# Attention and squared-ReLU MLP in one kernel: the softmax sums of three batches taken by block transposes and additions on VectorE, the last keys' product with v as two column tiles, and the second group of scores beside it

## The chip, the cores and the metric

The kernel runs on one core of one Trainium2 chip. The metric is the device time of one execution in microseconds (us), the median of several runs.

## The reference

Attention over q, k, v of shape (4 batches, 12 heads, 448 positions, 64), all float32, with capped scores, and then an MLP over the 4 x 448 tokens of width 768.

```python
scores = cap * np.tanh(scale * (q @ k.T) / cap)
attn = np.exp(scores - max);  attn = attn / (np.sum(attn, axis=-1, keepdims=True) + 1e-09)
x = (attn @ v).transpose(0, 2, 1, 3).reshape(4 * 448, 768)
h = x @ w_in                      # w_in (768, 2048)
r = np.maximum(h, 0.0)
g = s * (r * r) + b
y = g @ w_out                     # w_out (2048, 768)
```

## The kernel before

Work goes by pairs of heads: 24 pairs, six to a batch (PAIRS = 6, ALL = 24). For a pair everything is kept transposed, keys on the 128 partitions and the 448 queries along the free dimension. 448 keys are three full tiles of 128 (FULL = 3) and 64 left over. The left-over keys of both heads share one tile (AB): head 0 in its lower 64 partitions, head 1 in its upper ones. So e, the exponentials of a pair, is 7 tiles of 128x448.

TensorE, for a pair p: `first_scores(p)` makes four score tiles by four matmuls with 64 rows each (L249, two heads side by side as row tiles); `last_scores(p)` makes the AB tile by one whole-array matmul with a block-diagonal k (L258) and two row tiles (L261). `values(p)` multiplies e with v: first the AB tile with a block-diagonal v as one whole-array matmul that starts the accumulation (L272), then six matmuls of 64 output columns each (L277, column tiles, head 0 into PSUM partitions 0 to 63 and head 1 into 64 to 127). `sums(p)` multiplies the sum of the e tiles with a tile of ones, one column tile a head (L287): every partition of a head's half then holds that head's sum over keys. All these products are plain float32; the profile counts two records a matmul.

ScalarE makes e with `first_tanh`, `exponential`, `last_tanh`, `exponential` (L374 to L385). VectorE's `add_e(p)` adds the 7 tiles into e_sum (L465 to L472; two operations of 128x896 and two of 64x448). Its `scale_pair(p)` then waits for `sums(p)`, transposes the sums from PSUM in blocks of 32x32 (L479), adds the guard to one column a block (L481), inverts 14 numbers a partition (L484), spreads them back by a second block transpose (L486), multiplies with the product of `values(p)` (L490), and splits the result into a high and a low part (L495, L497), since the MLP's products run as three fp32r matmuls each (hi x hi, lo x hi, hi x lo).

There are three stages. First stage, pairs 0 to 5 (batch 0): attention only; TensorE runs `first_scores(p+1)`, `values(p)`, `last_scores(p+1)`, `sums(p)`. Two PSUM tensors, pv and hid, take turns (`pv_bank`). Second stage, periods 6 to 23: in period p TensorE does the scores of pair p+1, the values and sums of pair p, and between them 16 chunks (SHARE = 16) of the first MLP product of the batch before. A chunk (`hidden_chunk`, L306 to L308) is three matmuls; six chunks make one of 16 tiles of 128x448 in one of the two banks of hid. The order in a period is: first scores, 6 chunks, last scores, 2 chunks, values, sums, 8 chunks. Both values and sums of every pair use pv (bank 0 and bank 1). A tile is rectified by ScalarE (`rectify`, L395) into one of three slots of hidden_sb, squared by VectorE (`square`, L503), and stored by a DMA of queue SP (L182); rectify waits for the store three tiles before. Third stage: the last batch's first product and then all of the second product, `out_products`, L320 to L322; hidden tiles come back by DMA.

The weights w_in arrive in 24 pieces of 256 KB into a ring of four slots (`work`), each cast to fp32r by VectorE (`w_in_high`, L457) and its rest subtracted by GpSimd (L580). Twelve pieces are cast in the first stage, and three in each of periods 6 to 9. SP issues the loads of a period in program order with the stores and the loads of v and of q and k, and waits in that order too.

Of the kernel before, what the change touches and what calls it, by code (L numbers as in the profile page):

```python
# [7 lines left out]
ACT = mybir.ActivationFunctionType  # L8

# [26 lines left out]
BLOCK = 32  # L36
QK_SLOTS = 3
# [5 lines left out]
def attention_ffn(nc, q_k, v, cap, w_in, w_out, s, b, y_t):  # L43
    hidden = nc.dram_tensor("hidden_scratch", (B - 1, JT, P, S), F32).ap()
    ctx = ExitStack()
    with ctx:
# [20 lines left out]
        turned = sb("turned", [P, S], F32)  # L67
        r_sum = sb("r_sum", [P, S], F32)
        xt = sb("xt", [P, S], F32)
        recips = sb("recips", [P, 2, S // BLOCK], F32)  # L70
# [41 lines left out]
        sums_read = sem("sums_read")  # L112
        recip_done = sem("recip_done")
# [17 lines left out]
        def pv_bank(p):  # L131

            return hid if p < PAIRS and p % 2 else pv
# [22 lines left out]
        def _(sp):  # L156
# [46 lines left out]
            for p in range(PAIRS, ALL):  # L203
# [36 lines left out]
        def _(pe):  # L240
# [24 lines left out]
            def values(p):  # L265
                i, of = p % QK_SLOTS, p % 2
                out = pv_bank(p)
# [3 lines left out]
                reach(pe, x_done, p - 1 if p < PAIRS else p)  # L271
                nc.tensor.matmul(out[:, 0, 0:S], v_sb[:, i, 2 * FULL * D:], e[:, of, AB, :], start=True, stop=False)  # L272
                for t in range(FULL):
                    for head in range(2):
                        rows = slice(head * D, (head + 1) * D)
                        tile = (head * FULL + t) * D
                        last = nc.tensor.matmul(out[rows, 0, 0:S], v_sb[:, i, tile:tile + D], e[:, of, 2 * t + head, :],  # L277
                                                start=False, stop=t == FULL - 1)
                last.then_inc(pv_done, 1)

            def sums(p):
                out = pv_bank(p)
                pe.wait_ge(e_sum_done, 4 * (p + 1))
                reach(pe, sums_read, p - 1 if p < PAIRS else p)
# [54 lines left out]
            for p in range(PAIRS, ALL):  # L339
# [27 lines left out]
        def _(act):  # L367
# [51 lines left out]
            for p in range(PAIRS, ALL):  # L419
# [4 lines left out]
                for j in tiles_in(SHARE * c, SHARE * c + 6):  # L424
                    rectify((batch - 1) * JT + j)
# [3 lines left out]
                for j in tiles_in(SHARE * c + 6, SHARE * (c + 1)):  # L429
                    rectify((batch - 1) * JT + j)  # L430
# [22 lines left out]
        def _(dve):  # L453
# [7 lines left out]
            def add_e(p):  # L461
                of = p % 2
                dve.wait_ge(exp_done, 2 * p + 1)
                reach(dve, sums_done, p)
                nc.vector.tensor_tensor(e_sum[:], e[:, of, 0:2, :], e[:, of, 2:4, :], ALU.add).then_inc(e_sum_done, 1)  # L465
# [8 lines left out]

            def scale_pair(p):
                batch, c = divmod(p, PAIRS)
                out = pv_bank(p)
                dve.wait_ge(sums_done, p + 1)
                nc.vector.transpose(turned[:], out[:, 1, 0:S]).then_inc(sums_read, 1)  # L479
                dve.wait_ge(sums_read, p + 1)  # L480
                nc.vector.tensor_scalar(recips[:, 0, :], turned[:].rearrange("p (n i) -> p n i", i=BLOCK)[:, :, 0],  # L481
                                        guard_c, None, ALU.add).then_inc(recip_done, 1)
                dve.wait_ge(recip_done, 3 * p + 1)
                nc.vector.reciprocal(recips[:, 1, :], recips[:, 0, :]).then_inc(recip_done, 1)  # L484
                dve.wait_ge(recip_done, 3 * p + 2)
                nc.vector.transpose(r_sum[:], recips[:, 1, :].unsqueeze(2).broadcast_to([P, S // BLOCK, BLOCK])  # L486
# [123 lines left out]
```

## Time and profile before

| | |
|---|---|
| median of 3 runs | 677.98 us (677.97 to 678.04) |
| profiled execution | 678.0 us, span 676.2 us |
| TensorE busy | 663.9 us, 98% |
| VectorE busy | 282.3 us, 42% |
| ScalarE busy | 246.5 us, 36% |
| GpSimd busy | 33.4 us, 5% |
| granted TensorE clock | 1.00 (full, 2.4 GHz) |

The span runs from the first to the last instruction; the rest of the time lies around it. Busy time of TensorE counts a matmul until its modelled end, so a busy engine can still pass from one shape to another with small gaps: starts are the better measure. Idle time of an engine other than the one that sets the end costs nothing by itself.

### The profile page before, as it was taken

The page shows a single profiled execution, that of the slowest core. Times are in us where ns is not written, and L with a number is a line of the kernel's source. Part 1 is how long each engine was busy: PE and PEld are TensorE (multiplying, and loading weights), DVE is VectorE, ACT ScalarE, POOL GpSimd, SP SyncE. Part 2 cuts the span into 40 slices and gives each one's busy share as a digit, 9 for nine tenths or more (in the row PEclk, how much of TensorE's full clock was granted, in tenths as well). Part 3 has the DMA queues.
Part 4 walks back from the last instruction along what each step waited for, and adds up shares of the span by engine and source line. Part 5 has one row for each costly group of instructions (what it writes and reads, how often), then busy time and mean ns, then how long its engine had stood idle before and what let it go on. Part 6 is the DMA issues. An engine that isn't in the chain of part 4 may idle for free.

```text
span 676.2 us, 7857 instructions
## 1 busy us (share of the span) xinstructions
PE 663.9 (98%) x3122; PEld 500.0 (74%) x3122; DVE 282.3 (42%) x449; ACT 246.5 (36%) x255; POOL 33.4 (5%) x32
## 2 busy tenths in 40 slices
PE   7998999999999999999999999999999999999998
PEld 4332666666666666666667799999999999999997
DVE  3798744644445545545445343322431222212211
ACT  5777444444444444434442133222331121112110
POOL 2331222200000000000000000000000000000000
PEclk9999999999999999999999999999999999999999
DMA  7542134313213212221310331123152224215002
GB/s 221 167 142 91 44 103 145 100 57 98 83 57 98 83 57 85 86 67 47 100 51 36 118 94 47 50 68 113 31 190 69 59 77 138 56 41 178 1 0 82
DMA packets 38100, 57.93 MB, mean 86 GB/s; under 512 B 11440, under 2 KB 29872, under 8 KB 38064
## 3 DMA queue, kind: packets, MB, share of 16 engines
q1 hardware_dynamic: 37632, 57.43, 27.3%
q8 instruction: 25, 0.41, 0.3%
q14 instruction: 11, 0.09, 0.0%
q10 hardware_dynamic: 432, 0.00, 0.0%
HBM read 40.90 MB, written 16.52 MB: 85 GB/s over the span
## 4 chain that ended last, share of the span: by engine, by line
PE 96%; DVE 2%; ACT 1%; DMA 1%; issue 0%; SPq 0%; DVEq 0%
PE hid L306 13%; PE hid L307 12%; PE hid L308 12%; PE scores L321 8%; PE scores L320 8%; PE scores L322 8%; PE pv L277 7%; PE scores L249 6%; PE pv L321 4%; PE pv L322 4%; PE pv L320 4%; PE scores L261 3%; PE scores L258 3%; PE pv L272 2%; PE pv L287 2%; ACT e L379 1%
## 5 line engine op out<-in xcount | busy, mean ns | idle before, releaser
L306 PE MATMUL hid<-x_hi,w_hi 128*128 128x448 f32 x384 | 146.2, 381 | 0.6 <-DVE xt L490 0.6
L307 PE MATMUL hid<-x_lo,w_hi 128*128 128x448 f32 x384 | 140.5, 366 | 0.0
L308 PE MATMUL hid<-x_hi,w_lo 128*128 128x448 f32 x384 | 140.5, 366 | 0.0
L306 PEld LDWEIGHTS hid<-x_hi,w_hi 128*128 128x128 f32 x384 | 72.0, 188 | 40.8 <-issue 34.2
L320 PE MATMUL scores<-x_hi,w_hi 128*128 128x448 f32 x256 | 93.5, 365 | 0.0
L321 PE MATMUL scores<-x_lo,w_hi 128*128 128x448 f32 x256 | 93.5, 365 | 0.0
L322 PE MATMUL scores<-x_hi,w_lo 128*128 128x448 f32 x256 | 93.5, 365 | 0.0
L385 ACT ACTIVATE e<-e,const 128x1792 f32<-128x1792 f32 (+1 forms) x48 | 77.0, 1604 | 1.6
L308 PEld LDWEIGHTS hid<-x_hi,w_lo 128*128 128x128 f32 x384 | 72.1, 188 | 6.4
L307 PEld LDWEIGHTS hid<-x_lo,w_hi 128*128 128x128 f32 x384 | 72.2, 188 | 5.4
L508 DVE SCALAR_TENSOR_TENSOR x_lo<-e,const,x_hi 128x448 fp32r<-128x448 f32 x48 | 32.1, 683 | 103.8 <-ACT x_hi L399 103.8
L399 ACT ACTIVATE x_hi<-e,const 128x448 fp32r<-128x448 f32 x48 | 31.3, 669 | 104.5 <-PE pv L322 104.5
L395 ACT ACTIVATE hidden_sb<-hid 128x448 f32<-128x448 f32 x48 | 25.8, 537 | 117.8 <-PE hid L308 117.8
L374 ACT ACTIVATE e<-scores,const 128x1792 f32<-128x1792 f32 x24 | 42.2, 1758 | 44.4 <-PE scores L249 44.4
L479 DVE STREAM_TRANSPOSE turned<-pv 128x448 f32<-128x448 f32 x21 | 13.7, 651 | 95.2 <-PE pv L287 95.2
L277 PE MATMUL pv<-e,v_sb 128*64 128x448 f32 x252 | 52.0, 548 | 0.0
L320 PEld LDWEIGHTS scores<-x_hi,w_hi 128*128 128x128 f32 x256 | 48.1, 188 | 3.8
L321 PEld LDWEIGHTS scores<-x_lo,w_hi 128*128 128x128 f32 x256 | 48.1, 188 | 3.8
L322 PEld LDWEIGHTS scores<-x_hi,w_lo 128*128 128x128 f32 x256 | 48.1, 188 | 3.8
L503 DVE SCALAR_TENSOR_TENSOR hidden_sb<-hidden_sb,const 128x448 f32<-128x448 f32 x48 | 31.8, 683 | 44.8 <-ACT hidden_sb L395 44.3
L249 PE MATMUL scores<-qk 64*128 64x448 f32 x192 | 42.6, 561 | 5.1 <-ACT e L379 4.8
L320 PE MATMUL pv<-x_hi,w_hi 128*128 128x448 f32 x128 | 46.7, 365 | 0.0
(63 smaller groups left out, 658.4 us busy)
## 6 DMA issues: line engine op xcount, KB each, us to landing
qk<-q_k SPq DMA_DIRECT2D x24, 448.0 KB, 3.3
hidden_scratch<-hidden_sb SPq DMA_DIRECT2D x48, 224.0 KB, 1.9
e<-hidden_scratch SPq DMA_DIRECT2D x48, 224.0 KB, 2.6
work<-w_in SPq DMA_DIRECT2D x24, 256.0 KB, 4.1
e<-w_out SPq DMA_DIRECT2D x16, 384.0 KB, 3.1
y_t<-qk SPq DMA_DIRECT2D x24, 224.0 KB, 2.0
v_sb<-v SPq DMA_DIRECT2D x24, 192.0 KB, 2.5
k_ab<-q_k SPq DMA_DIRECT2D x48, 16.0 KB, 3.1
```

Source lines behind the costliest of these rows:

```text
L249: last = nc.tensor.matmul(scores[:, 2 * t + head, 0:S], qk[rows, i, 1, t * P:(t + 1) * P], qk[rows, i, 0, :], start=True, stop=True)
L277: last = nc.tensor.matmul(out[rows, 0, 0:S], v_sb[:, i, tile:tile + D], e[:, of, 2 * t + head, :], start=False, stop=t == FULL - 1)
L306: nc.tensor.matmul(out, w_hi[:, j, w], x_hi[:, batch % 2, c, :], start=c == 0, stop=False)
L307: nc.tensor.matmul(out, w_hi[:, j, w], x_lo[:, batch % 2, c, :], start=False, stop=False)
L308: last = nc.tensor.matmul(out, w_lo[:, j, w], x_hi[:, batch % 2, c, :], start=False, stop=c == CT - 1)
L320: nc.tensor.matmul(y_acc(c), w_hi[:, j, w], ring(x_hi, n), start=j == 0, stop=False)
L321: nc.tensor.matmul(y_acc(c), w_hi[:, j, w], ring(x_lo, n), start=False, stop=False)
L322: last = nc.tensor.matmul(y_acc(c), w_lo[:, j, w], ring(x_hi, n), start=False, stop=j == JT - 1)
L374: nc.scalar.activation(e[:, of, 0:G1, :], scores[:, 0:G1, 0:S], ACT.Tanh, scale=tanh_scale).then_inc(tanh_done, 1)
L385: nc.scalar.activation(e[:, p % 2, tiles, :], e[:, p % 2, tiles, :], ACT.Exp, scale=cap_c).then_inc(exp_done, 1)
L503: nc.vector.scalar_tensor_tensor(r, r, s_c, r, ALU.mult, ALU.mult).then_inc(sq_done, 1)
L508: nc.vector.scalar_tensor_tensor(ring(x_lo, n), source, b_c, ring(x_hi, n).bitcast(F32), ALU.add, ALU.subtract).then_inc(g_lo_done, 1)
```

## The change

In the second stage the sums are no longer a matmul. VectorE transposes e_sum in blocks of 32x32 (128x896), sums each block's 32 elements (a reduction to 28 numbers a partition), brings the four groups of 32 partitions beside each other by one guarded addition and three copies, sums those, inverts, copies the results back to four groups of partitions, and spreads them by a last block transpose as before. `invert(p)` for pair p stands a period earlier than the multiplication, behind `scale_pair(p-1)`. The first stage keeps the matmuls with ones (`invert_first`). In all pairs the AB tile's product with v becomes two column tiles (64 columns of the block-diagonal v each, all 128 rows), last in `values`, so that the whole-array matmul is gone. In the second stage the products of successive pairs take turns on the two banks of pv, and `values(p)` waits for x of pair p-1. The order in a period becomes: first scores, 8 chunks, last scores, values, 8 chunks. `add_e` is cut in two, the first addition standing before the squares. SP issues the loads of v and of q and k ahead of the period's stores.

```diff
         def pv_out(p):
+            return first_banks(p)[:, 0, 0:S] if p < PAIRS else pv[:, p % 2, 0:S]
...
@@ sync, period p
-                for j in tiles_in(SHARE * c, SHARE * c + 8):
-                    store_hidden((batch - 1) * JT + j)
                 if p + 2 < ALL:
                     load_v(p + 2)
-                for j in tiles_in(SHARE * c + 8, SHARE * (c + 1)):
-                    store_hidden((batch - 1) * JT + j)
                 if p + 3 < ALL:
                     load_qk(p + 3)
+                for j in tiles_in(SHARE * c, SHARE * (c + 1)):
+                    store_hidden((batch - 1) * JT + j)
...
@@ tensor, values(p)
-                reach(pe, x_done, p - 1 if p < PAIRS else p)
-                nc.tensor.matmul(out[:, 0, 0:S], v_sb[:, i, 2 * FULL * D:], e[:, of, AB, :], start=True, stop=False)
-                for t in range(FULL):
+                reach(pe, x_done, p - 1)
+                for t in range(FULL + 1):
                     for head in range(2):
                         rows = slice(head * D, (head + 1) * D)
-                        tile = (head * FULL + t) * D
-                        last = nc.tensor.matmul(out[rows, 0, 0:S], v_sb[:, i, tile:tile + D], e[:, of, 2 * t + head, :],
-                                                start=False, stop=t == FULL - 1)
+                        tile = (head * FULL + t) * D if t < FULL else (2 * FULL + head) * D
+                        of_e = 2 * t + head if t < FULL else AB
+                        last = nc.tensor.matmul(out[rows], v_sb[:, i, tile:tile + D], e[:, of, of_e, :],
+                                                start=t == 0, stop=t == FULL)
...
@@ tensor, period p
-                for chunk in range(SHARE * c, SHARE * c + 6):
+                for chunk in range(SHARE * c, SHARE * c + 8):
                     hidden_chunk(batch - 1, chunk)
                 if p + 1 < ALL:
                     last_scores(p + 1)
-                for chunk in range(SHARE * c + 6, SHARE * c + 8):
-                    hidden_chunk(batch - 1, chunk)
                 values(p)
-                sums(p)
                 for chunk in range(SHARE * c + 8, SHARE * (c + 1)):
                     hidden_chunk(batch - 1, chunk)
...
@@ scalar, period p: rectify before the last tanh for tiles up to chunk 8 of the period, not 6
...
@@ vector
+            def invert(p):
+                m = p - PAIRS
+                dve.wait_ge(e_sum_done, 4 * (p + 1))
+                nc.vector.transpose(turned[:].rearrange("p h s -> p (h s)"), e_sum[:].rearrange("p h s -> p (h s)")
+                                    ).then_inc(turned_done, 1)
+                dve.wait_ge(turned_done, m + 1)
+                nc.vector.tensor_reduce(parts[:], turned[:].rearrange("p h (n i) -> p (h n) i", i=BLOCK), AX.X, ALU.add
+                                        ).then_inc(parts_done, 1)
+                dve.wait_ge(parts_done, m + 1)
+                nc.vector.tensor_scalar(quads[:, 0, :], parts[0:BLOCK, :], guard_c[0:BLOCK], None, ALU.add
+                                        ).then_inc(quads_done, 1)
+                for k in range(1, P // BLOCK):
+                    nc.vector.tensor_copy(quads[:, k, :], parts[k * BLOCK:(k + 1) * BLOCK, :]).then_inc(quads_done, 1)
+                dve.wait_ge(quads_done, P // BLOCK * (m + 1))
+                nc.vector.tensor_reduce(totals[:, 0, :], quads[:].rearrange("p k n -> p n k"), AX.X, ALU.add
+                                        ).then_inc(totals_done, 1)
+                dve.wait_ge(totals_done, m + 1)
+                nc.vector.reciprocal(totals[:, 1, :], totals[:, 0, :]).then_inc(inverse_done, 1)
+                dve.wait_ge(inverse_done, 2 * PAIRS + m + 1)
+                for k in range(P // BLOCK):
+                    head = k * BLOCK // D
+                    nc.vector.tensor_copy(recips[k * BLOCK:(k + 1) * BLOCK, 0, :],
+                                          totals[:, 1, head * BLOCKS:(head + 1) * BLOCKS]).then_inc(spread_done, 1)
+                dve.wait_ge(spread_done, P // BLOCK * (m + 1))
+                nc.vector.transpose(r_sum[:], recips[:, 0, :].unsqueeze(2).broadcast_to([P, BLOCKS, BLOCK])
+                                    ).then_inc(recip_done, 1)
...
@@ vector, period p
-                for j in tiles_in(SHARE * c, SHARE * c + 6):
-                    square((batch - 1) * JT + j)
                 if batch == 1 and c < 4:
                     for piece in range(12 + 3 * c, 15 + 3 * c):
                         w_in_high(piece)
+                if p + 1 < ALL:
+                    add_first_e(p + 1)
+                for j in tiles_in(SHARE * c, SHARE * c + 8):
+                    square((batch - 1) * JT + j)
+                if p + 1 < ALL:
+                    add_last_e(p + 1)
                 scale_pair(p)
                 if p + 1 < ALL:
-                    add_e(p + 1)
-                for j in tiles_in(SHARE * c + 6, SHARE * (c + 1)):
+                    invert(p + 1)
+                for j in tiles_in(SHARE * c + 8, SHARE * (c + 1)):
                     square((batch - 1) * JT + j)
```

## Rows read from the trace of the kernel before

**Rows 1.** Page: busy time of each engine, and granted clock in 40 slices.
```profile
PE 663.9 (98%) x3122; PEld 500.0 (74%) x3122; DVE 282.3 (42%) x449; ACT 246.5 (36%) x255; POOL 33.4 (5%) x32
...
PEclk9999999999999999999999999999999999999999
```

**Rows 2.** Page: the chain that ended last, shares by engine.
```profile
PE 96%; DVE 2%; ACT 1%; DMA 1%; issue 0%; SPq 0%; DVEq 0%
```

**Rows 3.** Timeline, PE: start us, us, line, count, over one pair.
```profile
207.69 1.77 PE L249 MATMUL scores<-qk 64*128 64x448 f32 x8
...
213.15 0.91 PE L258 MATMUL scores<-qk,k_ab 128*128 128x448 f32 x2
213.99 1.02 PE L261 MATMUL scores<-qk 64*128 64x448 f32 x4
214.95 0.47 PE L306 MATMUL hid<-x_hi,w_hi 128*128 128x448 f32 x1
215.25 0.36 PE L307 MATMUL hid<-x_lo,w_hi 128*128 128x448 f32 x1
...
216.27 0.91 PE L272 MATMUL pv<-e,v_sb 128*128 128x448 f32 x2
217.11 2.48 PE L277 MATMUL pv<-e,v_sb 128*64 128x448 f32 x12
219.42 0.92 PE L287 MATMUL pv<-e_sum,ones 128*64 128x448 f32 x4
220.27 0.47 PE L306 MATMUL hid<-x_hi,w_hi 128*128 128x448 f32 x1
220.58 0.36 PE L307 MATMUL hid<-x_lo,w_hi 128*128 128x448 f32 x1
...
225.42 1.77 PE L249 MATMUL scores<-qk 64*128 64x448 f32 x8
```

**Rows 4.** Timeline, PE: one pair of the first stage.
```profile
48.03 1.77 PE L249 MATMUL scores<-qk 64*128 64x448 f32 x8 [0.67 <-ACT e L379]
49.73 1.02 PE L272 MATMUL pv<-e,v_sb 128*128 128x448 f32 x2
50.68 2.48 PE L277 MATMUL pv<-e,v_sb 128*64 128x448 f32 x12
53.09 1.02 PE L258 MATMUL scores<-qk,k_ab 128*128 128x448 f32 x2
...
54.99 0.97 PE L287 MATMUL pv<-e_sum,ones 128*64 128x448 f32 x4
56.63 1.77 PE L249 MATMUL scores<-qk 64*128 64x448 f32 x8 [0.67 <-ACT e L379]
```

**Rows 5.** Timeline, DVE: the guard of the fifth pair.
```profile
56.69 1.02 DVE L481 TENSOR_SCALAR recips<-turned,const 128x14 f32<-128x14 f32 x1
```

**Rows 6.** Timeline, PE: end of the first stage.
```profile
63.97 0.97 PE L287 MATMUL hid<-e_sum,ones 128*64 128x448 f32 x4 [0.31 <-DVE e_sum L472]
...
67.59 0.47 PE L306 MATMUL hid<-x_hi,w_hi 128*128 128x448 f32 x1 [0.58 <-DVE xt L490]
```

**Rows 7.** Groups of DVE by line and shape: count, busy us, mean ns.
```profile
L472 DVE TENSOR_TENSOR e_sum<-e_sum,e 64x448 f32<-64x448 f32 x48 | 29.8, 620 | 1.6
...
L465 DVE TENSOR_TENSOR e_sum<-e 128x896 f32<-128x896 f32 x24 | 26.0, 1085 | 0.0
L486 DVE STREAM_TRANSPOSE r_sum<-recips 128x448 f32<-128x448 f32 x24 | 15.5, 645 | 0.8
...
L484 DVE RECIPROCAL recips<-recips 128x14 f32<-128x14 f32 x24 | 5.8, 241 | 0.8
```

**Rows 8.** Busy time in one window of the second stage.
```profile
185.00:385.00 200.00, 200.00 (x910) 134.22 (x910) 98.03 (x159) 79.18 (x72) 0.00 (x0) 1.00 0.22 70
```

**Rows 9.** Timeline, DVE: a cast that waits for its weights.
```profile
114.28 0.43 DVE L457 CAST w_hi<-work 128x512 fp32r<-128x512 f32 x1 [5.72 <-DMA work<-w_in]
```

**Rows 10.** Page: DMA issues, KB each, median us to landing.
```profile
work<-w_in SPq DMA_DIRECT2D x24, 256.0 KB, 4.1
```

More of the change, by code:

```diff
@@ L8 @@
 ACT = mybir.ActivationFunctionType
+AX = mybir.AxisListType
 B, H, S, D = 4, 12, 448, 64
@@ L36 @@
 BLOCK = 32
+BLOCKS = S // BLOCK
 QK_SLOTS = 3
@@ L112, in attention_ffn @@
         sums_read = sem("sums_read")
+        turned_done = sem("turned_done")
+        parts_done = sem("parts_done")
+        quads_done = sem("quads_done")
+        totals_done = sem("totals_done")
+        inverse_done = sem("inverse_done")
+        spread_done = sem("spread_done")
         recip_done = sem("recip_done")
@@ L129, in reach, with first_banks, pv_out @@
                 eng.wait_ge(semaphore, n)
-        def pv_bank(p):
-            return hid if p < PAIRS and p % 2 else pv
+        def first_banks(p):
+            return hid if p % 2 else pv
+        def pv_out(p):
+            return first_banks(p)[:, 0, 0:S] if p < PAIRS else pv[:, p % 2, 0:S]
         def tiles_in(first, last):
@@ L459, in w_in_high, with add_first_e, add_last_e @@
                                       ).then_inc(w_in_hi, 1)
-            def add_e(p):
+            def add_first_e(p):
+                dve.wait_ge(exp_done, 2 * p + 1)
+                if p <= PAIRS:
+                    reach(dve, sums_done, p)
+                else:
+                    dve.wait_ge(turned_done, p - PAIRS)
+                nc.vector.tensor_tensor(e_sum[:], e[:, p % 2, 0:2, :], e[:, p % 2, 2:4, :], ALU.add
+                                        ).then_inc(e_sum_done, 1)
+            def add_last_e(p):
                 of = p % 2
-                dve.wait_ge(exp_done, 2 * p + 1)
-                reach(dve, sums_done, p)
-                nc.vector.tensor_tensor(e_sum[:], e[:, of, 0:2, :], e[:, of, 2:4, :], ALU.add).then_inc(e_sum_done, 1)
                 dve.wait_ge(exp_done, 2 * p + 2)
@@ L473, in add_e, with invert_first @@
                                             ).then_inc(e_sum_done, 1)
+            def invert_first(p):
+                dve.wait_ge(sums_done, p + 1)
+                nc.vector.transpose(turned[:, 0, :], first_banks(p)[:, 1, 0:S]).then_inc(sums_read, 1)
+                dve.wait_ge(sums_read, p + 1)
+                nc.vector.tensor_scalar(recips[:, 0, :], turned[:, 0, :].rearrange("p (n i) -> p n i", i=BLOCK)[:, :, 0],
+                                        guard_c, None, ALU.add).then_inc(inverse_done, 1)
+                dve.wait_ge(inverse_done, 2 * p + 1)
+                nc.vector.reciprocal(recips[:, 1, :], recips[:, 0, :]).then_inc(inverse_done, 1)
+                dve.wait_ge(inverse_done, 2 * p + 2)
+                nc.vector.transpose(r_sum[:], recips[:, 1, :].unsqueeze(2).broadcast_to([P, BLOCKS, BLOCK])
+                                    ).then_inc(recip_done, 1)
@@ L484, in scale_pair @@
-                nc.vector.reciprocal(recips[:, 1, :], recips[:, 0, :]).then_inc(recip_done, 1)
-                dve.wait_ge(recip_done, 3 * p + 2)
-                nc.vector.transpose(r_sum[:], recips[:, 1, :].unsqueeze(2).broadcast_to([P, S // BLOCK, BLOCK])
-                                    ).then_inc(recip_done, 1)
-                dve.wait_ge(recip_done, 3 * p + 3)
+                dve.wait_ge(recip_done, p + 1)
                 dve.wait_ge(pv_done, p + 1)
-                nc.vector.tensor_tensor(xt[:], out[:, 0, 0:S], r_sum[:], ALU.mult).then_inc(x_done, 1)
+                nc.vector.tensor_tensor(xt[:], pv_out(p), r_sum[:], ALU.mult).then_inc(x_done, 1)
```

33 lines of the change are left out of this document (17 added, 16 removed).

## Prediction

> **What bounds the kernel now.** I read the page first. TensorE is busy for 663.9 of 676.2 us and the granted clock is full in all 40 slices [rows 1]; VectorE has 42%, ScalarE 36%. The chain of work that ended last is TensorE for 96% and VectorE for 2% [rows 2]. So nearly every microsecond that leaves TensorE's queue leaves the kernel, and everything else costs nothing until it makes TensorE wait. Second, the timeline of TensorE over one pair of the second stage [rows 3]. From one L249 to the next it takes 225.42 - 207.69 = 17.73 us, with no idle time in front of any row. The differences of the starts are what each piece costs: 0.84 us for the whole-array product L258 or L272, 0.96 for the two row tiles L261, 2.31 for the six column tiles L277 (0.77 for each two of them, one per head, side by side), 0.85 for the two column tiles with ones, L287. The first matmul of a chunk behind tiles takes 0.30 or 0.31 (214.95 to 215.25, 220.27 to 220.58), where one amid chunks takes about 0.20 (six of them fill 214.95 to 216.27 with that first one: (1.32 - 0.30) / 5). So there is a toll of some 0.1 us on leaving a shape of tile and another 0.1 on entering the next: a switch costs about 0.2 us. Third, the first stage [rows 4 to 6], where TensorE and ScalarE take turns and VectorE comes close. Last, the groups of VectorE by shape and its share of a quiet window [rows 7, 8].
>
> **TensorE in the second stage, pairs 6 to 22.** Before, L258 to the second matmul of the chunk behind L261 is 215.25 - 213.15 = 2.10 us, and L272 to the second matmul behind the sums is 220.58 - 216.27 = 4.31, together 6.41 [rows 3]. After: L258 0.84 and L261 0.95 (they now run straight into column tiles; the same 0.95 or so as before a chunk), then four times two column tiles. Three times two cost 2.31, and the fourth two, the last keys', stand where the sums stood and end as they did: 0.85 + 0.31. The whole-array L272 is gone. That is 0.84 + 0.95 + 2.31 + 0.85 + 0.31 = 5.26, and the first matmul of the chunk that used to stand behind the scores is now an ordinary one, 0.20: 5.46. The saving is 6.41 - 5.46 = 0.95 us a pair: 0.75 for one pass of 448 columns in fp32 fewer, and 0.20 for one switch fewer (six a period become five). 17 x 0.95 = 16.2 us. The last pair (23) has no scores beside it; a pass goes and no switch does: 0.75. Sum for the stage: 16.9 us.
>
> The Trainium skill, TensorEngine Tiling (Array Packing), Key Properties, says that changing the mode of tiling, not just the tile, drains TensorE; the 0.84 of L272 against a pass of about 0.75 and the 0.31 of the first chunk matmul agree. By that rule the move of the scores gains, by a count of passes alone it would not.
>
> **The first stage, pairs 0 to 5.** The sums stay there, on the same two banks. Only the last keys' product changes: L272 and L277 together take 53.09 - 49.73 = 3.36 us, L272 0.95 of it [rows 4]; four times two column tiles take 2.41 + 0.75 = 3.16. Row tiles now run straight into column tiles. The loop is first scores, values, last scores, ScalarE's tanh over them, first scores again (0.67 idle for it at 56.63), so each pair gains 0.20 while nothing else binds: 1.2 us. VectorE nearly binds: at 63.97 L287 has waited 0.31 for its additions, and the first chunk at 67.59 has waited 0.58 for x, which hangs on that L287 [rows 6], in the pair where the guard op took 1.02 us [rows 5] although the reciprocal of that size takes 0.24 [rows 7], so 0.78 of it is a block. From L287's end (54.99 + 0.97) to the next L287 VectorE needs 63.97 - 55.96 = 8.01, 7.2 without the block; with L287 that is 8.2 us a loop against TensorE's 56.63 - 48.03 = 8.60 before and 8.40 after [rows 4]. If the block stays in the fifth pair, the stage gains 0.8; if the shifted times dissolve it, 0.78 more, about 1.5. I take 1.1.
>
> **VectorE.** Per pair of the second stage it loses the transpose of the sums (0.65) and, replaced in kind, the guard, the reciprocal and the last transpose (0.24 + 0.24 + 0.65): 1.8 us. The new chain has 12 instructions. Transpose of 128x896: between 0.65 (the row for half the size) and twice that; I take 1.12, as 448 elements more cost an addition 1.09 - 0.62 = 0.47 [rows 7]. The reduction of 128x896 is shown by no row; its bounds are 0.65 and four times 1.09, and I take the addition of that shape, 1.09. Guard, three copies, small reduction, reciprocal and four copies, ten ops on 28 to 112 elements: between nothing (hidden in the op before) and 0.27 each with the gap; I take 0.26, 2.6 us. The last transpose 0.65. Sum 5.5 us, bounds 2 and 9. The transposes and the chain are off TensorE's path: values(p) no longer waits for anything of its own sums, only for x of the pair before. VectorE's busy time per period is now 98.03 x 17.73 / 200 = 8.7 us [rows 8] and becomes 8.7 - 1.8 + 5.5 = 12.4 of 16.8.
>
> The Trainium skill, VectorE: DVE Perf Modes, Rules for kernel authors, speaks against this part: it calls a reduction the slowest VectorE op, sends reductions across partitions to GpSimd and asks for fewer ops. Its tier table (2.29 us for 2048 fp32 elements at the lowest rate) gives an estimate of 1.00 us for 896. No run so far shows the op. By the rule alone VectorE could become the bound; that is the third rival.
>
> **What is queued behind the chain.** The adds of pair p+1 now wait for ScalarE ahead of scale_pair(p), the new chain follows, and only then the squares of the period's last tiles, their stores (SP) and SP's next loads. While w_in still loads (periods 6 to 9) this closes a loop: SP issues one piece only behind the last store of the period before, the third cast of the period waits for it (it waited 5.72 us already [rows 9]; landing takes 4.1 [rows 10]), and the chain and the squares follow. I count 4.1 + 0.6 for issuing + 0.43 for the cast + 12.4 = 17.5 us against a period of 16.8: VectorE falls back by about 0.7 us in each of three such loops. By adding the pieces up from 66.5 us on, the square behind the chain comes about 12 us after its matmuls in period 7 and 16 to 17 in period 9; from period 10 no piece is waited for and VectorE catches up. Who waits? ScalarE's rectify of tile n needs the store of tile n-3, three tiles being 18 chunks or 16.8 x 18 / 16 = 18.9 us; with a landing of at most 4.1 that is 17 + 4.1 - 18.9 = 2 us late for ScalarE, once. TensorE needs the rectified tile only a tile (6 us) later, since hid has two banks: 4 us of cover left. Hence no stall, cost 0. Without that cover the cost is the lag itself. The earlier issue of v and q_k loads and the later stores lie under two periods of slack: 0. At the end of a batch chunk 5 of the next one needs x of the last pair, 12 us after the scores; scale_pair is through 7 us after them: 0. The third stage is untouched and its own chain to w_out starts from the same last square: 0.
>
> **Sum.** 16.2 + 0.75 + 1.1 = 18.0 us. The profiled execution took 678.0 us, 1.8 of it outside the span of 676.2; the median of the runs is 677.98, the same. So the span becomes 658.2 and the time 660.0 us.
>
> **Rivals.** (1) Switches are not saved: row tiles into column tiles cost as much as going by way of a chunk, and the first stage gains nothing. Then 18 x 0.75 = 13.5 us, 664.5 us. Against it: in the first stage L261 runs straight into L287, and L287 comes to 0.97 there with both tolls in it. Chance 0.08. (2) The lag of VectorE in the periods with w_in reaches TensorE. With the small ops at their upper end and blocked by GpSimd's subtractions, like the guard in rows 5, each loop would lose 2.5 to 4 us instead of 0.7; the 4 us of cover are gone by period 9, and the rest, 3 x 2.6 - 4 = 4 us, comes back as waits at the chunks that start a tile: 664. Chance 0.12. (3) VectorE becomes the bound in every period, and the kernel is slower. To lose, VectorE must need more than 17.73 + 0.1 us a period, so the new chain more than 17.8 - 6.9 = 10.9 us; with a reduction at four additions (4.4), twice 0.65 for the transpose, 0.65 and ten small ops at 0.46 it gets there, and at 11.5 the period is 18.4 and the time 678.0 + 18 x 0.67 - 1.1 = 689.0. Against it: no small op of the trace is near 0.46 without a block. Chance 0.02. (4) The two column tiles of the last keys don't run side by side, since both stream the same tile of e: each pair costs a pass (0.75) more, 17 x 0.2 = 3.4 us gained and 6 x 0.55 = 3.3 lost in the first stage: 677.9, no change. Against it: L277's twos overlap fully, and nothing in rows 3 depends on what is streamed. Chance 0.03. (5) Better than the sum, 657.5: the block in the first stage goes and chunks behind tiles run a little closer. Chance 0.04.
>
> **How the numbers follow.** My forecast has 0.71, and its own range is 658.8 to 661.8 (the first stage's 0.8 to 1.5, and 0.05 us a pair either way). The range for 8 in 10 reaches up to rivals 1 and 2 and down by the same uncertainty: 658.0 to 664.2. A measurement can tell about 0.2%, 1.4 us, from no change. Faster by more than that: forecast, 1, 2 and 5, 0.95; within it: 4, 0.03; slower: 3, 0.02.
>
> **What would show it.** Right: a period of 16.78 us between L249s in the second stage, L258, L261 and four twos of column tiles in a row without idle time, six switches become five; VectorE busy 12 us a period; no wait of TensorE for relu or x_done; the chunks of the second stage otherwise as before. Wrong: a wait of TensorE at L306 (now L320) for ScalarE's rectify, itself waiting for a store, around period 9 (rival 2); 0.2 us of idle time in front of column tiles (rival 1); a reduction well over 1.1 us or periods of over 17 us that end on VectorE (rival 3).

## The result and the profile after

The changed kernel takes 658.1 us (median of 4 runs, 657.97 to 658.21) against 678.01 beside it: a ratio of 0.970, interval 0.969 to 0.971. The forecast was 660.0, with an own range of 658.8 to 661.8 and a wider one of 658.0 to 664.2: the time came 1.9 us lower, below the first and at the very edge of the second. The profiled execution took 658.2, its span 656.4.

The page of the changed kernel: busy time by engine, granted clock in 40 slices, and the chain that ended last by engine.

```profile
PE 644.7 (98%) x3098; PEld 494.9 (75%) x3098; DVE 339.0 (52%) x611; ACT 247.2 (38%) x255; POOL 36.7 (6%) x32
...
PEclk9999999999999999999999999999999999999999
...
PE 94%; DVE 4%; ACT 1%; issue 1%; DVEq 0%
```

TensorE's busy time fell by 19.2 us, the span by 19.8, and the chain is still TensorE's [rows 1, 2]. The clock was full throughout.

TensorE in one period of the second stage (timeline: start, us, line, count; L262 is the first scores, L271 and L274 the last ones, L291 the values, L320 to L322 a chunk):

```profile
198.12 1.77 PE L262 MATMUL scores<-qk 64*128 64x448 f32 x8
...
204.79 0.92 PE L271 MATMUL scores<-qk,k_ab 128*128 128x448 f32 x2
205.64 1.02 PE L274 MATMUL scores<-qk 64*128 64x448 f32 x4
206.59 3.23 PE L291 MATMUL pv<-e,v_sb 128*64 128x448 f32 x16
209.75 0.47 PE L320 MATMUL hid<-x_hi,w_hi 128*128 128x448 f32 x1
210.05 0.36 PE L321 MATMUL hid<-x_lo,w_hi 128*128 128x448 f32 x1
...
214.51 0.36 PE L322 MATMUL hid<-x_hi,w_lo 128*128 128x448 f32 x1
214.81 1.40 PE L262 MATMUL scores<-qk 64*128 64x448 f32 x6
```

A period is 214.81 - 198.12 = 16.69 us; the forecast was 16.78, and before it was 17.73 [rows 3]. The pieces are those of the forecast: 0.85, 0.95, 3.16 for four twos of column tiles (forecast 2.31 + 0.85), 0.30 for the first chunk matmul. The 23 matmuls from 210.05 on lie (214.51 - 210.05) / 22 = 0.2027 us apart. Before, the same 23 behind the sums were 0.2064 apart: between 220.58 and 225.42 lie 23 of them and the entry into the first scores, 4.84 us [rows 3]; here that stretch is 214.81 - 210.05 = 4.76. That is the missing 0.09, to rounding. I call the time from one such start to the next the pace of a run of equal matmuls; a two is a couple of column tiles that run side by side, one per head.

The end of the first stage (TensorE's timeline), and VectorE's guard op of the fifth pair:

```profile
54.53 0.97 PE L301 MATMUL pv<-e_sum,ones 128*64 128x448 f32 x4 [0.25 <-DVE e_sum L490]
...
62.73 0.97 PE L301 MATMUL hid<-e_sum,ones 128*64 128x448 f32 x4
...
66.34 0.47 PE L320 MATMUL hid<-x_hi,w_hi 128*128 128x448 f32 x1 [0.31 <-DVE xt L539]
```
```profile
56.24 0.23 DVE L498 TENSOR_SCALAR recips<-turned,const 128x14 f32<-128x14 f32 x1
```

The second stage starts at 66.34 and not at 67.59 [rows 6]: 1.25 us. The guard op that took 1.02 [rows 5] takes 0.23 here: in this pair the block is gone (one of the six, at 30.66, still takes 1.22, in the third pair as before). L301 of the last pair starts 1.24 earlier, and the first chunk waits 0.31 instead of 0.58. From the first stage's end to the first chunk behind the last pair it is 289.98 us (66.34 to 356.32) where it was 308.51 (67.59 to 376.10): 18.53. What is left behind that point is 300.1 us in both. 1.25 + 18.53 = 19.8: the whole difference.

VectorE: its new operations (groups by line and shape: count, busy us, mean ns), its busy time in a window of the second stage, and the one place where ScalarE waits for a store:

```profile
L509 DVE STREAM_TRANSPOSE turned<-e_sum 128x896 f32<-128x896 f32 x18 | 19.9, 1105 | 0.0
L513 DVE TENSOR_REDUCE parts<-turned 128x28 f32<-128x896 f32 x18 | 19.5, 1086 | 0.6
...
L529 DVE COPY recips<-totals 32x14 f32<-32x14 f32 x72 | 12.0, 166 | 2.3
...
L519 DVE COPY quads<-parts 32x28 f32<-32x28 f32 x54 | 9.1, 169 | 1.7
L521 DVE TENSOR_REDUCE totals<-quads 32x28 f32<-32x112 f32 x18 | 6.2, 343 | 0.6
L524 DVE RECIPROCAL totals<-totals 32x28 f32<-32x28 f32 x18 | 5.7, 316 | 0.6
```
```profile
184.00:366.00 182.00, 182.00 (x858) 125.90 (x857) 120.92 (x241) 78.81 (x71) 0.00 (x0) 1.00 0.23 75
```
```profile
129.15 0.55 ACT L406 ACTIVATE hidden_sb<-hid 128x448 f32<-128x448 f32 x1 [3.05 <-DMA hidden_scratch<-hidden_sb]
```

The transpose of 128x896 took 1.10 us and the reduction 1.09 (1.12 and 1.09 were taken). Seven copies took 0.17 each, and by the timeline 0.57 for three and 0.76 for four, so that some 0.03 lies between two of them. From the transpose's start (197.01) to the end of the last one (202.31) the chain is 5.3 us, 5.5 forecast. Busy per period: 120.92 x 16.69 / 182 = 11.1 us, 12.4 forecast. That window reaches 10 us beyond the stage; over the seven whole periods from 198.12 to 314.92 it is 79.91 / 7 = 11.4. ScalarE waited 3.05 us for a store, once, in period 9; the forecast said 2, once, there.

### The profile page after: what moved, and what is told of

Its sections match the earlier page's. It is cut to its first block, busy times and chain, and to the rows that moved or that the text cites. A ratio compares the mean times of both kernels' runs of the same rounds, so it can differ in the third digit from the quotient of the medians.

```text
span 656.4 us, 7953 instructions
## 1 busy us (share of the span) xinstructions
PE 644.7 (98%) x3098; PEld 494.9 (75%) x3098; DVE 339.0 (52%) x611; ACT 247.2 (38%) x255; POOL 36.7 (6%) x32
## 4 chain that ended last, share of the span: by engine, by line
PE 94%; DVE 4%; ACT 1%; issue 1%; DVEq 0%
PE hid L320 13%; PE hid L322 12%; PE hid L321 12%; PE pv L291 9%; PE scores L334 8%; PE scores L335 8%; PE scores L336 8%; PE scores L262 5%; PE pv L334 4%; PE pv L335 4%; PE pv L336 4%; PE scores L274 3%; PE scores L271 2%; PE pv L344 1%; DVE e_sum L490 1%; DVE e_sum L486 1%
## 5 line engine op out<-in xcount | busy, mean ns | idle before, releaser
L320 PE MATMUL hid<-x_hi,w_hi 128*128 128x448 f32 x384 | 143.9, 375 | 0.3 <-DVE xt L539 0.3
L322 PE MATMUL hid<-x_hi,w_lo 128*128 128x448 f32 x384 | 140.3, 365 | 0.0
L320 PEld LDWEIGHTS hid<-x_hi,w_hi 128*128 128x128 f32 x384 | 72.1, 188 | 29.3 <-issue 23.1
L322 PEld LDWEIGHTS hid<-x_hi,w_lo 128*128 128x128 f32 x384 | 72.1, 188 | 5.7
L291 PE MATMUL pv<-e,v_sb 128*64 128x448 f32 x336 | 67.8, 545 | 0.0
L291 PEld LDWEIGHTS pv<-e,v_sb 128*64 128x64 f32 x336 | 22.2, 136 | 42.6 <-issue 42.6
L486 DVE TENSOR_TENSOR e_sum<-e_sum,e 128x896 f32<-128x896 f32 x24 | 26.2, 1090 | 46.8 <-ACT e L396 46.2
L390 ACT ACTIVATE e<-scores,const 128x1344 f32<-128x1344 f32 x24 | 33.2, 1382 | 44.3 <-PE scores L274 44.3
L552 DVE SCALAR_TENSOR_TENSOR work<-work,const 128x448 f32<-128x448 f32 x16 | 11.0, 685 | 70.0 <-ACT work L406 70.0
```

The source lines that it names most:

```text
L291: last = nc.tensor.matmul(out[rows], v_sb[:, i, tile:tile + D], e[:, of, of_e, :], start=t == 0, stop=t == FULL)
L320: nc.tensor.matmul(out, w_hi[:, j, w], x_hi[:, batch % 2, c, :], start=c == 0, stop=False)
L322: last = nc.tensor.matmul(out, w_lo[:, j, w], x_hi[:, batch % 2, c, :], start=False, stop=c == CT - 1)
L390: nc.scalar.activation(e[:, p % 2, G1:TILES, :], scores[:, 0:G2, 0:S], ACT.Tanh, scale=tanh_scale).then_inc(tanh_done, 1)
L486: nc.vector.tensor_tensor(e_sum[:], e_sum[:], e[:, of, 4:6, :], ALU.add).then_inc(e_sum_done, 1)
```

## The experiments

The kernel before took 678.0 to 678.1 us beside all of them. In some executions TensorE's clock is at its lower level for part of the first of the page's 40 slices, which adds some 2.4 us to any of these kernels; where a median mixes both, the time at the full clock is given too.

### The parts by themselves, and the sums put back

**Column tiles only** (a1_cols): in the kernel before, `values` as in the changed kernel.

```diff
-                nc.tensor.matmul(out[:, 0, 0:S], v_sb[:, i, 2 * FULL * D:], e[:, of, AB, :], start=True, stop=False)
-                for t in range(FULL):
+                for t in range(FULL + 1):       # the last keys as t == FULL, two column tiles
...
```

> The kernel before with only the last keys' product with v as two column tiles; sums and order as before. Theory of passes and switches: in the second stage nothing is gained (a whole-array pass becomes a pass of two column tiles, and the switch whole array to column tiles only moves from behind it to in front of it), in the first stage 0.2 us a pair and the dissolved block of the guard op: 1.2 to 1.4 us, so 676.7. Beside it the chunks behind values, 0.2064 us a matmul before and 0.2027 in the changed kernel, worth 1.6 us in all. If the whole-array product in front of the column tiles makes them slow (S1), they are fast here: 675.0. If the sums do (S2) or the place of the scores does (S3), they stay slow: 676.7.

Measured: 682.1, at the full clock 680.8 and 680.9: slower than before by 2.8, where no theory expected it. The period was 17.64 and not 17.73, the 23 matmuls behind the sums ran at 0.2027, and the second stage began at 66.22: all as S1 said. But the second product, from its first to its last matmul, took 286.2 us instead of 280.7.

**Order only** (a2_order): in the kernel before, eight chunks, last scores, values, sums, eight chunks.

```diff
-                for chunk in range(SHARE * c, SHARE * c + 6):
+                for chunk in range(SHARE * c, SHARE * c + 8):
                     hidden_chunk(batch - 1, chunk)
                 if p + 1 < ALL:
                     last_scores(p + 1)
-                for chunk in range(SHARE * c + 6, SHARE * c + 8):
-                    hidden_chunk(batch - 1, chunk)
                 values(p)
...                                             # rectify and square of the tiles moved with the chunks
```

> The kernel before with only the order changed: eight chunks, last scores, values, sums, eight chunks (rectify and square moved with it). The tiles of the scores now run into the whole-array L272, so the number of switches stays six: 678.0 by passes and switches. A gain of 3.4 us would say that the scores beside the values save a switch by themselves. S1 and S2: chunks behind the sums stay at 0.2064. S3 (the place of the scores decides): 0.2027 and 676.4.

Measured: 676.6, at the full clock 676.4 to 676.7; period 17.64, and the 23 matmuls at 0.2023 to 0.2027. So the order by itself saves no switch (not the 3.4 us), but the pace changed, as S3 said: 17 x 0.09 = 1.5 us.

**Sums only** (a3_sums): the changed kernel with L272 and the old order back.

> The changed kernel with the whole-array product L272 and the old order put back, so that of the change only the sums on VectorE are left. One pass of 0.76 us a pair goes, 18 x 0.76 = 13.7: 664.3. S2 (the sums make the chunks slow): they are fast and it is 662.7. S1 and S3: slow, 664.3. Rival 2 and 3 (VectorE's chain costs time): more than 665 with waits in TensorE's queue.

Measured: 664.2; the two executions at the full clock 662.9 and 663.2. Period 16.89. The pace is the fast one here too. It is what S2 said, and S2 falls by the run before, where the sums were there and the pace was fast. From the forecast's terms: 18 x 0.75 = 13.5 for the pass, 1.5 for the pace: 663.0.

**An unused pass in place of the sums** (a4_dummy): in the changed kernel, behind `values`.

```diff
                 values(p)
+                if p == ALL - 1:
+                    pe.wait_ge(tanh_done, 2 * ALL)
+                for head in range(2):
+                    rows = slice(head * D, (head + 1) * D)
+                    nc.tensor.matmul(scores[rows, G1 - 1, 0:S], ones[:], e[:, p % 2, head, :], start=True, stop=True)
```

> The changed kernel with two unused column tiles of ones times e behind the values of each second-stage pair, into a free bank of scores: the pass of the sums is back, its result not used. 18 x 0.77 = 13.9 us more than the changed kernel, 672.0. S2: the chunks behind them are slow again, 673.6. S1 and S3: fast, 672.0.

Measured: 680.3, at the full clock 679.2. Period 17.53 = 16.69 + 0.75 + 0.09, the 23 matmuls at 0.2064, and the second product 286.2 us. Without the two effects of the pace (1.6 and 5.5) it would be the expected 672. So two more column tiles cost 21 us here, 7 of them by the pace.

**One switch** (a5_whole): the changed kernel with the whole-array product in front of six column tiles, 0.95 us in place of the 0.75 of two column tiles.

> The changed kernel with the last keys' product with v as one whole-array matmul again, in front of six column tiles; sums on VectorE and the new order kept. Passes are equal in number, so this is the price of one switch: row tiles to whole array to column tiles (0.95 us for the whole-array matmul by the rows of the kernel before) in place of row tiles to column tiles. Theory: 0.20 us x 17 in the second stage, 1.2 to 1.4 in the first, 658.1 + 4.7 = 662.8. Rival 1 (switches cost nothing to speak of): 658 to 659.

Measured: 663.0 (662.8 to 663.1 at the full clock), 4.9 over the changed kernel; period 16.88, 0.19 more. The switch is worth what the forecast said, and the first stage too.

### What sets the pace of the whole-array matmuls

S1, S2 and S3 are all refuted: each named one part, and the four runs above show the pace fast and slow with and without it. The pace in force when TensorE leaves the last pair's column tiles holds for the 300 us behind them. In the kernel with column tiles only, the page's group of the second product's first matmul (count, busy us, mean ns):

```profile
L321 PE MATMUL scores<-x_hi,w_hi 128*128 128x448 f32 x256 | 94.2, 368 | 0.0
...
L321 PE MATMUL pv<-x_hi,w_hi 128*128 128x448 f32 x128 | 47.1, 368 | 0.0
```

against 365 before and in the changed kernel. To see whether it is really the way out of the tiles, two small row tiles (64 columns, unused) were put behind the last pair's sums of that kernel:

```diff
                 sums(p)
+                if p == ALL - 1:
+                    pe.wait_ge(tanh_done, 2 * ALL)
+                    for head in range(2):
+                        rows = slice(head * D, (head + 1) * D)
+                        nc.tensor.matmul(scores[:, head, 0:D], qk[rows, p % QK_SLOTS, 1, 0:P],
+                                         qk[rows, p % QK_SLOTS, 0, 0:D], start=True, stop=True)
```

> The kernel with only the column tiles for the last keys, and behind the last pair's sums two small unused row tiles (64 columns each), so that TensorE enters its last long run of whole-array matmuls from row tiles and not from column tiles. Without them that run (first to last matmul of the second product) took 286.2 us, with 0.2064 us a matmul, where it takes 280.7 in the kernel before. Theory: the pace of a run of whole-array matmuls is set by how the array left its tiles, and holds until the next switch; from row tiles it has always been the fast one. Then the second product takes 280.7 again and the time falls by 5.5 us less about 0.3 for the tiles: 675.7 to 677. Rival: the slow last stage has another cause (operands, DMA, memory), and it stays at 286 and above 681.

Measured: 675.5, 5.4 less than 680.9. The same group:

```profile
L321 PE MATMUL scores<-x_hi,w_hi 128*128 128x448 f32 x256 | 93.5, 365 | 0.0
```

Two matmuls that do nothing save 5.4 us. The rival (operands, DMA) is out. That it takes row tiles to do it is not shown by this run: further down a single small whole-array matmul turns the pace as well, and it can turn it either way. So the column tiles alone, with a good way out, gain 2.6 us on the kernel before: 1.4 in the first stage and 1.5 by the pace, less 0.3 for the two tiles.

A section of TensorE work alone (m1_modes) behind the changed kernel tried 30 patterns, results unused:

```python
# in outline
row_tiles();  whole(between)                  # 0, 6 or 48 fp32r matmuls, 128x128 by 448
if fp32_whole: one whole-array fp32 matmul
column_tiles(n);  whole(24)                   # n = 1 to 5 twos of column tiles; then the 24 that are read
```

> The changed kernel with a section of TensorE work alone behind it, its results unused: 30 times row tiles, then 0, 6 or 48 whole-array fp32r matmuls, then none or one whole-array fp32 matmul, then one to five twos of column tiles, then 24 fp32r matmuls, whose spacing is read; and three runs of column tiles and 24 whole-array matmuls six times in turn without row tiles between. Theory 1 (parity): the number of twos of column tiles, odd or even, decides between 0.2027 and 0.2064 us, whatever stands before. Theory 2 (history): the pace before counts too, and in the runs without row tiles it alternates. Theory 3 (waits): the pace hangs on semaphores or other engines, and with TensorE alone all of it runs at 0.2027. The section adds about 30 x 11 + 18 x 8 = 470 us.

Measured: 21 of the 30 runs of 24 took 5.12 or 5.13 us and 9 took 5.21 or 5.22: there are two paces and nothing between. Two patterns of the timeline (row tiles, column tiles, the 24):

```profile
681.71 1.77 PE L385 MATMUL pv<-x_hi,w_hi 64*128 64x448 f32 x8
683.41 3.23 PE L392 MATMUL hid<-x_hi,w_hi 128*64 128x448 f32 x16
686.57 5.13 PE L379 MATMUL hid<-x_hi,w_hi 128*128 128x448 f32 x24
691.63 1.77 PE L385 MATMUL pv<-x_hi,w_hi 64*128 64x448 f32 x8
693.33 3.98 PE L392 MATMUL hid<-x_hi,w_hi 128*64 128x448 f32 x20
697.24 5.21 PE L379 MATMUL hid<-x_hi,w_hi 128*128 128x448 f32 x24
```

From 660 us on no other engine is busy and TensorE has no waits, and both paces occur, so theory 3 is out. Parity is out as well: five twos gave the slow pace behind row tiles and the fast one behind row tiles and six matmuls. In the turns without row tiles the pace did not alternate: three twos were fast throughout, four twos slow once and then fast, five twos fast twice and then slow. The simple form of theory 2 is out.

A second section (m2_place) repeated one pattern (row tiles, four twos, 24 whole) 36 times, with small matmuls put in or the 24 made longer:

> The changed kernel with another section of TensorE work alone behind it: 36 times row tiles, four twos of column tiles and 24 whole-array fp32r matmuls, 12 times identically, 12 times with 0 to 3 small matmuls (64 columns) in front, 12 times with 24 to 35 whole-array matmuls. Theory A (pattern): what stands before decides, and the first 12 are alike. Theory B (place in the instruction stream or in time): the slow pace (0.2065 against 0.2026 us) comes and goes among identical repeats, and shifts with the number of matmuls put in.

Measured: of the 12 identical repeats the first was fast and the other eleven slow (5.21 or 5.22). The one behind them, with no small matmul in front either, was slow too (779.12). Two of the repeats with one matmul of 64 columns (L403) in front, and the one just ahead of the second of them:

```profile
779.12 5.22 PE L379 MATMUL hid<-x_hi,w_hi 128*128 128x448 f32 x24
784.17 0.19 PE L403 MATMUL hid<-x_hi,w_hi 128*128 128x64 f32 x1
...
789.16 5.13 PE L379 MATMUL hid<-x_hi,w_hi 128*128 128x448 f32 x24
...
819.32 5.13 PE L379 MATMUL hid<-x_hi,w_hi 128*128 128x448 f32 x24
824.29 0.19 PE L403 MATMUL hid<-x_hi,w_hi 128*128 128x64 f32 x1
...
829.27 5.22 PE L379 MATMUL hid<-x_hi,w_hi 128*128 128x448 f32 x24
```

One small matmul ahead of the row tiles turned the slow pace into the fast one (789.16), and four and eight repeats later the same small matmul turned it back (829.27, and 869.48, not shown). With two or three in front the repeats were fast. With 24 to 28 whole matmuls they stayed fast, with 29 to 35 they were slow. So what stands just before does not decide. Theory B is nearer, but it is open whether something is carried from one repeat to the next or the place in the program or in time counts: each repeat stands at another place, so these runs can't separate the two. Changing the number of matmuls by one can turn the pace.

What is shown is that there are two paces, 2% apart, and that a pace can last for 300 us. In the kernels it was nearly always chosen at a change of tiling. Behind column tiles it depended on the kernel: slow in 17 of 18 stretches before, in 18 of 18 in a4_dummy, in none of 18 in the changed kernel. Behind row tiles it was fast in 203 of the 205 stretches of 18 or more matmuls in the second stage of these kernels (c1_reset's last run among them). The two others were at 0.2065, in b1_two from 68.61 and in d1_sp from 121.88. And once it changed within a run: in b1_two a matmul of a run that began at 175.22 started 0.03 us late (at 178.40) and was followed after 0.28 us instead of 0.20, and from there a matmul took 368 ns on average and not 365. So in this one case a small hitch did it, without a change of tiling.

### How much cover VectorE has

Two and five more reductions of 128x896 in each pair's chain (repeats that leave the sums as they are):

```diff
+                for r in range(2):              # b2_five: 5
+                    dve.wait_ge(parts_done, 3 * m + r + 1)
+                    nc.vector.tensor_reduce(parts[:], turned[:]..., AX.X, ALU.add).then_inc(parts_done, 1)
```

> The changed kernel with two more reductions of 128x896 in every pair's chain on VectorE (repeats, 2 x 1.12 = 2.2 us a pair). Theory (VectorE off the path, with cover): busy 11.1 + 2.2 = 13.3 of 16.7 us a period, the lag behind TensorE in the periods with w_in grows from some 10 us by 2.2 a period, ScalarE may wait for a store, TensorE hardly: 658 to 661. Rival 2: TensorE already has no cover left there: each of four periods loses 2 us, 666.

Measured: 665.9; the two executions with the full clock in the first slice took 664.4 and 664.9, 6.3 and 6.8 over the changed kernel: nearer to rival 2. TensorE waited once in the second stage, 4.3 us, for the rectified tile, and the clock fell behind it. The windows of the period around the wait and of the next (the number behind POOL's is the granted clock):

```profile
130.00:146.60 16.60, 12.28 (x52) 9.74 (x51) 12.80 (x24) 6.25 (x6) 4.68 (x3) 0.90 0.29 88
146.60:163.20 16.60, 16.60 (x78) 10.90 (x77) 15.88 (x29) 6.02 (x6) 0.00 (x0) 1.00 0.22 69
```

130.0 to 146.6 has 0.90 of the clock on average, which is 1.7 us: behind the wait the starts of some nine matmuls lie 0.37 us apart and not 0.20. With the 4.3 that makes 6.0 of the 6.3 to 6.8. If each of three loops put its 2.25 us on top of the last, 6.8 were sent and 4.3 arrived; by this estimate the cover was 2.5 us, not the 4 that the forecast counted. In the changed kernel's trace GpSimd's subtractions (4.94 us of three in a row from 76.59 on) block three VectorE ops in period 6 (1.53 us for a cast that takes 0.43, 2.17 for an addition of 1.09, 1.70 for a square of 0.68), as in rows 5: some lag is there before the first loop.

> The same with five more, 5.6 us a pair: busy 16.7 of 16.7 us a period, 18.5 with the casts. Theory: VectorE is now at the bound; in the periods with w_in the lag grows by over 6 us each and TensorE waits for rectified tiles, some 12 to 20 us in all, and behind them nothing is won back: 670 to 680. If it stays under 662, VectorE has more cover than I count.

Measured: 698.2, beyond the 680. TensorE's waits in that kernel (us, times, longest):

```profile
PE hid L320 <- ACT hidden_sb L406: 18.2, 5, 6.9
PE hid L320 <- DVE x_lo L550: 9.8, 3, 3.5
```

28 us of waits, and a granted clock of 0.983 over a span of 696 us, which is 12 us more: together the 40 over the changed kernel. The second wait (for x of a new batch) was not among the waits that I expected here; the prediction had looked at it and put it at 0 for a chain of half this length. The chain is 5.3 + 5 x 1.12 = 10.9 us, the length from which rival 3 saw the kernel lose, and it does lose. But it loses by eight waits and the clock behind them, four of them between 105 and 176 us; between 208 and 258 us the periods are still 16.69 us. VectorE as the bound of every period did not occur in any run.

### SP's order, and who was queued behind whom

**SP's old order** (d1_sp) in the changed kernel: stores of the first tiles, load of v, other stores, load of q and k.

> The changed kernel with SP's old order of stores and loads in a period. Theory: loads of v, q and k have two periods of slack either way, 658.1 (within 0.5). Rival: the earlier loads carry part of the gain, 659 or more.

Measured: 666.0 (665.4 to 670.1): 7.9 slower. The rival holds. SP in that kernel, and TensorE at the start of period 9's first scores (L264):

```profile
115.16 0.33 SPq L197 DMA_DIRECT2D hidden_scratch<-hidden_sb  x1
115.53 0.43 SPq L176 DMA_DIRECT2D qk<-q_k  x1
116.01 0.47 SPq L177 DMA_DIRECT2D k_ab<-q_k  x1
```
```profile
119.55 2.40 PE L264 MATMUL scores<-qk 64*128 64x448 f32 x8 [2.50 <-DMA k_ab<-q_k]
```

SP issued q and k for pair 10 at 115.53, behind a store that waited for a square behind the chain; TensorE wanted them at 117.05 and got them at 119.55, and the clock fell again (0.90 from 110 to 127). It happened three times in the second stage, with waits of 2.50, 1.44 and 2.20, 6.1 us in all (a fourth wait for k_ab, 0.72 us, stands at 6.43, and the kernel of the next experiment has it too). Behind the first and the third the clock was lower for a while, which added some 3 us in this profiled execution (670.1); behind the second it stayed full. In the changed kernel SP issues q and k of the same pair ahead of the period's stores:

```profile
95.96 0.58 SPq L176 DMA_DIRECT2D qk<-q_k  x1
...
99.41 10.73 SPq L197 DMA_DIRECT2D hidden_scratch<-hidden_sb  x3
```

at 95.96, 20 us earlier, and 3 us ahead of the first store.

**Squares ahead of the chain, SP's old order** (e1_squares):

```diff
                 scale_pair(p)
-                if p + 1 < ALL:
-                    invert(p + 1)
                 for j in tiles_in(SHARE * c + 8, SHARE * (c + 1)):
                     square((batch - 1) * JT + j)
+                if p + 1 < ALL:
+                    invert(p + 1)
```

> SP's old order as in the run before (d1_sp, 666.0 us, TensorE waiting four times for q and k), but the squares of a period's last tiles stand ahead of the chain of the sums on VectorE. Theory: the loads of q and k came late only because they were queued behind stores that waited for squares behind the chain; with the squares first the waits for q and k go and the time is that of the changed kernel, 658.1 within 1. Rival: SP's order itself costs the time (queueing of the loads behind other transfers): 665 or more.

Measured: 658.12 (658.0 to 658.3), no waits of TensorE in the second stage, with SP's old order. The order of the transfers by itself costs nothing; the place of the chain in VectorE's queue made them late. Either repair is enough.

## Why the prediction was right or wrong

**Right: the mechanism and its terms.** One pass fewer: a4_dummy put it back at 0.75 a pair, a3_sums took it away for 0.75. One switch fewer: 0.19 a pair by a5_whole against 0.20, and no gain by the order alone, as the count of six switches said. L271 to L291 run without idle time. The Trainium skill, TensorEngine Tiling (Array Packing), Key Properties, says that a change of the mode of tiling drains TensorE, without a price; the 0.19 agrees with it.

**Mis-sized: the sum for the second stage.** The terms "17 x 0.95 = 16.2 us" and 0.75 for the last pair, 16.9 together, measured 18.53, 1.6 more (1.04 a pair and not 0.95). The step that failed is the one behind it, "the chunks of the second stage otherwise as before": the 23 matmuls behind the column tiles went from 0.2064 to 0.2027 us, 0.09 us a pair over 18 pairs. The prediction put this term at nothing, without a reason. The row was there before the run: 220.58 to 225.42 in rows 3 holds them, and I took 0.20 for a chunk matmul from the stretch in front of the values and never divided this one. Had I seen two paces I could not have forecast which one the new order would get: a2_order, a3_sums and a5_whole got the fast one, a4_dummy the slow one. So 1.6 us of the gain are luck: with the slow pace the sum would have been right to 0.3 us, and with the slow pace for the last run too, as in a4_dummy, the kernel would have come out 5 to 6 us above it.

**The first stage**: 1.25 against 1.1, within its bounds of 0.8 and 1.5. The block of the fifth pair dissolved, as the upper end had it; TensorE's first scores began 0.08 us later at the start and the second ones 0.17.

**VectorE**: the chain 5.3 against 5.5, the reduction at the price of an addition. The Trainium skill, VectorE: DVE Perf Modes, Rules for kernel authors, calls it the slowest op; at 128x896 the trace has 1.086 us for it and 1.090 for the addition, so here it is not slower. The same table sends a sum across partitions to GpSimd; no run here tried that, and with the block transposes in front VectorE did it without costing TensorE a wait.

**Wrong though without effect on the sum: two statements of cover.** The cover in the periods with w_in was 2.5 us and not 4, by the estimate from b1_two. And "the earlier issue of v and q_k loads ... lie under two periods of slack: 0" priced the edit of SP's order at nothing. For the changed kernel no wait appeared, but with the old order beside the new chain it is 7.9 us (d1_sp); the slack is there because of that edit, or would be by putting the squares ahead of the chain (e1_squares). I checked the new order and not what the old one would do beside the new chain.

**The rivals.** 1 (no switch saved) is refuted by a5_whole. 2 did not occur, and by that estimate it stood 2.5 us away. 3 did not occur either; b2_five, with twice the chain, is slower than the kernel before. 4 is refuted: four twos take 3.16 us. 5 named "chunks behind tiles run a little closer" and the dissolved block, at 0.04 and 657.5; that is what happened.

## What to carry to other kernels

Divide each long run of equal matmuls in the trace by its count, stretch by stretch: a pace that differs by 2% behind one kind of tile is a term of its own, and a cheap matmul at a change of tiling can turn it for all that follows. Which way it turns could not be foretold here, so measure the last long run of each variant before comparing two of them. When work moves to an engine with spare time, follow its queue through the others (here squares, stores, and SP's loads of q and k) and price an edit of the order by what happens without it. Count a wait of TensorE of some us for more than itself if the clock can fall behind it.

## What the runs showed of the hardware

Whole-array fp32r matmuls of 448 columns ran at either 0.2026 or 0.2065 us from start to start, in the kernels and with TensorE alone. In a1_cols the slow pace, once chosen on leaving column tiles, held for 302 us, to the last matmul. On leaving row tiles it was fast in 203 of 205 stretches, and slow in one of b1_two and one of d1_sp; in b1_two it also changed once without a change of tiling. What chooses it is open. A change of tiling cost 0.19 us (a5_whole). Behind waits of TensorE of 4.3 us (b1_two) and 2.5 us (d1_sp) the granted clock of the window fell to 0.90 on average, and in the stretch at the lower level the matmuls lay 0.37 us apart. On VectorE at 128x896 in fp32 a reduction took 1.086 us, an addition 1.090 and a transpose in blocks of 32x32 1.105.
